# One fused attention, FFN and mixture-of-experts kernel: TensorE's program for the FFN chunks written straight instead of as a loop, and half of chunk 0's first product placed ahead of unit 4's transposes

## What is computed

```python
q_s = softmax(q, axis=-1);  k_s = softmax(k, axis=2)          # 8 x 8 heads, 576 x 64 each
x = q_s @ (k_s^T v)                                           # -> x: 4608 x 512
h = x @ w_in;  g = h - tanh(h);  x = g @ w_out                # 512 -> 2048 -> 512
logits = norm(x) @ norm(expert_emb).T / tau;  e = argmax(logits)
out = softmax(logits)[e] * (relu(x @ w1[e]) @ w2[e])          # 512 -> 1024 -> 512, by token
```

## Time and profile before

| | |
|---|---|
| median of 3 runs | 1433.05 us (1432.52 to 1435.44) |
| the profiled execution's own time | 1435.76 us |
| its span, first to last instruction | 1433.8 us |
| PE busy | 1411.8 us, 98% |
| DVE, ACT, POOL busy | 905.3, 767.2, 393.4 us |
| stages in the span | opening with chunks 0 to 15 to about 118 us; loop of slots 16 to 159 to 820.85 us; slots 160 to 191 to about 957 us; expert tiles to the end |

### The profile page before, as it was taken

How to read it: one execution, slowest core, us unless ns; L and a number is a source line. 1 busy time by engine, 2 the same in 40 slices (tenths; PEclk the granted TensorE clock), 3 DMA queues, 4 the chain that set the end, 5 groups by cost and what they waited for, 6 DMA issues and landing times.

```text
span 1433.8 us, 27060 instructions
## 1 busy us (share of the span) xinstructions
PE 1411.8 (98%) x8124; PEld 1218.9 (85%) x8125; DVE 905.3 (63%) x1761; ACT 767.2 (54%) x1574; POOL 393.4 (27%) x345
## 2 busy tenths in 40 slices
PE   7999999999999999999999999999999999999997
PEld 5888888888888888888888888888888888888886
DVE  7996888886688887578888666676323313342221
ACT  6876576766566575657676666663324223242221
POOL 4422343532243433325343323221000000001000
PEclk9999999999999999999999999999999999999999
DMA  9632022121012122002121002035411411501110
GB/s 233 179 75 65 2 72 50 50 50 50 1 48 51 52 46 51 24 1 73 30 68 26 23 1 82 0 104 170 164 44 43 155 44 33 168 29 51 44 35 33
DMA packets 132387, 90.32 MB, mean 63 GB/s; under 512 B 107160, under 2 KB 113048, under 8 KB 132128
## 3 DMA queue, kind: packets, MB, share of 16 engines
q1 hardware_dynamic: 126128, 69.49, 18.5%
q0 software_dynamic: 5840, 18.92, 3.4%
q10 hardware_dynamic: 288, 0.33, 0.1%
HBM read 69.80 MB, written 21.28 MB: 64 GB/s over the span
## 4 chain that ended last, share of the span: by engine, by line
PE 94%; DVE 2%; issue 1%; POOL 1%; ACT 1%; DMA 0%; SPq 0%; POOLq 0%; DVEq 0%; ACTq 0%
PE ps L586 28%; PE ps L587 28%; PE ps L588 28%; PE ps L803 2%; PE ps L680 2%; PE ps L772 1%; PE ps L702 1%; PE ps L686 1%; PE ps L691 1%; PE ps L722 1%; PE ps L672 0%; PE ps L643 0%; DMA q_sb<-q 0%; DVE wo_lo L1260 0%; DVE gs L1112 0%
## 5 line engine op out<-in xcount | busy, mean ns | idle before, releaser
L1550 POOL TENSOR_TENSOR g_lo<-gs,g_hi 128x384 fp32r<-128x384 f32 x191 | 195.0, 1021 | 568.2 <-ACT g_hi L908 568.0
L586 PE MATMUL ps<-x_hi,wi_hi 128*128 128x384 f32 x768 | 277.9, 362 | 1.2 <-issue 1.2
L587 PE MATMUL ps<-x_lo,wi_hi 128*128 128x384 f32 x768 | 260.0, 339 | 0.0
L588 PE MATMUL ps<-x_hi,wi_lo 128*128 128x384 f32 x768 | 259.9, 338 | 0.0
L896 ACT ACTIVATE usq<-ps 128x384 f32<-128x384 f32 x192 | 94.1, 490 | 287.1 <-PE ps L588 286.6
L586 PE MATMUL ps<-wo_hi,g_hi 128*128 128x512 f32 x570 | 225.7, 396 | 1.9 <-issue 1.9
L587 PE MATMUL ps<-wo_lo,g_hi 128*128 128x512 f32 x570 | 226.7, 398 | 0.0
L588 PE MATMUL ps<-wo_hi,g_lo 128*128 128x512 f32 x570 | 225.0, 395 | 0.0
L1109 DVE SCALAR_TENSOR_TENSOR gs<-gs,ps 128x384 f32<-128x384 f32 x192 | 105.9, 551 | 145.2 <-ACT gs L903 144.0
L1360 DVE TENSOR_TENSOR t_lo<-ps,t_hi 128x512 fp32r<-128x512 f32 x37 | 25.6, 691 | 242.6 <-ACT t_hi L998 238.2
L1112 DVE TENSOR_TENSOR gs<-gs,usq 128x384 f32<-128x384 f32 x192 | 171.6, 894 | 0.0
(11 more groups left out here) (225 smaller groups left out, 2700.0 us busy)
## 6 DMA issues: line engine op xcount, KB each, us to landing
w_raw<-w SPq DMA_DIRECT2D x10, 2048.0 KB
xrow<-scratch SPq DMA_DIRECT2D x36, 257.0 KB, 2.7
v_sb<-v SPq DMA_DIRECT2D x60, 144.0 KB, 3.4
k_sb<-k SPq DMA_DIRECT2D x56, 144.0 KB, 3.4
q_sb<-q SPq DMA_DIRECT2D x56, 144.0 KB, 3.2
in_raw<-w_in SPq DMA_DIRECT2D x8, 512.0 KB, 6.1
out_raw<-w_out SPq DMA_DIRECT2D x8, 512.0 KB, 5.8
scratch<-pad_d SPq DMA_DIRECT2D x8, 257.0 KB, 4.2
```

The lines of the kernel that those rows point to most:

```text
L586: mm(out_, a_hi, b_hi, start=first, stop=False)
L587: mm(out_, a_hi, b_lo, start=False, stop=False)
L588: return mm(out_, a_lo, b_hi, start=False, stop=last)
L1550: G.tensor_tensor(g_lo[:, (s - 1) % 3], gs[:, (s - 1) % 2], g_hi[:, (s - 1) % 3].bitcast(F32), ALU.subtract).then_inc(glo_ready, 1)
```

## The change

It has two parts, both in PE's stream alone.

1. A new item `early:0` stands in PE's order between `out:3` and `qa:4`. It runs the first product of chunk 0 for its first two groups of three matmuls (`SOONER`, units 0 and 1), waiting only for the x of units 0 and 1 and the first split piece of `w_in`. `chunk:0` then runs the other two groups (`LATER`).
2. PE no longer goes through `walk`. Slots 15 to 191 are written out one after the other, with constants in every wait. The other four engines keep their loops.

```diff
-        "qa:3 kv:3 qb:3 out:2 kT:4 out:3 qa:4 row:4 chunk:0 kv:4 qb:4 chunk:1 out:4 chunk:2 kT:5 chunk:3 "
+        "qa:3 kv:3 qb:3 out:2 kT:4 out:3 early:0 qa:4 row:4 chunk:0 kv:4 qb:4 chunk:1 out:4 chunk:2 kT:5 chunk:3 "
...
+SOONER, LATER = (0, 1), (2, 3)
...
-        def first_product(m, s):
+        def first_product(m, s, pieces=range(DC)):
...
-                pe.wait_ge(xlo_b, m * 8 + (UPB if blk == 0 else 2 * UPB) + 1)
+                units = UPB if blk == 0 else 2 * UPB
+                pe.wait_ge(xlo_b, m * 8 + units + 1 if DC - 1 in pieces else len(pieces) + 1)
...
-            pe.wait_ge(g_ready, done(m, s, -2))
+            if 0 in pieces:
+                pe.wait_ge(g_ready, done(m, s, -2))
...
-            for dc in range(DC):
+            for dc in pieces:
...
-            last.then_inc(h_ready, 1)
+            if DC - 1 in pieces:
+                last.then_inc(h_ready, 1)
...
+            if what == "early":
+                first_product(0, 0, SOONER)
+                return
...
-            first_product(0, c)
+            first_product(0, c, LATER if c == 0 else range(DC))
...
-        walk(pe, slot, {SUPER - 1: first_rows_T})
+        for c in range(FILL, NCH):
+            if c == NCH - 1:
+                first_rows_T()
+            slot(c // SUPER, c % SUPER)
```

## The result

The changed kernel takes 1429.97 us in the median of 16 runs (1428.25 to 1432.03). The kernel before, run beside it, takes 1433.85 us (16 runs, 1431.55 to 1436.75). The ratio is 0.9971, 95% interval 0.9964 to 0.9978: 0.29% less time, about 4.1 us, where 4.0 us (0.28%) were forecast. The forecast 1429.05 us started from 1433.05 us; the kernel before now has 0.8 us more, and the changed kernel 0.9 us more. The span fell from 1433.8 to 1429.8 us.

A forecast was written before the change was run, and what follows sets the result against it. The prediction took PE, busy 98% of the span, to bound the kernel. Its terms, -4.09 + 0.2 - 0.1 = -4.0 us, took 1433.05 us to 1429.05 us, 0.28% less, range 1427.9 to 1431.3 us.

The forecast's parts named there:

- The loop on PE: At the FFN loop's two back-branches on PE: writing the loop straight removes the stalls, -4.09 us.
- What is late next: Behind ACT's own back-branch: POOL's piece comes late and PE waits 0.1 us at each, +0.2 us (0 to 2.26).
- The early matmuls: Six matmuls ahead of unit 4's transposes: PE's 1.1 us lead is mostly lost to DVE, -0.1 us.
- The kept lead: Rival, opening: PE keeps the early matmuls' 1.1 us lead, 1428.1 us; chance 0.08.
- ACT's branch taking over: Rival, FFN back-branches: ACT's full 1.13 us lateness reaches PE at each, 1.9 us gained, 1431.1 us; chance 0.13.
- Removal of the stalls: Rival, straight FFN stream on PE: the change moves the stalls and does not remove them, about 1433 us; chance 0.06.
- The expert loop did not begin to fetch: Rival claimed the opposite: PE's expert loop begins to fetch, 2.04 us at each of six back-branches, 1441.3 us; chance 0.08.

The follow-up runs named there:

- straight tiles: The changed kernel with PE's expert loop (7 turns of 4 tiles) written straight too; ratio 0.9967 to the kernel before.
- All engines straight: The changed kernel with slots 15 to 191 written straight for ACT, DVE and POOL too; ratio 0.9960 to the kernel before.
- early only: The kernel before with half of chunk 0's first product ahead of unit 4's transposes, PE's loop kept; ratio 0.9999 to the kernel before.
- turn of 12 tiles: The changed kernel with PE's expert loop as 4 tiles straight, then 2 turns of 12 tiles, 2020 instructions each; ratio 0.9997 to the kernel before.
- loop four slots later: The kernel before with PE's FFN loop over slots 20 to 163 instead of 16 to 159, same body length; ratio 1.0015 to the kernel before.
- straight only: The kernel before with PE's FFN program written straight and no matmuls moved in the opening; ratio 0.9963 to the kernel before.

## Why the prediction was right

**The loop on PE, -4.09 us.** Right: the middle gained 4.11 us in the changed kernel. The experiments give the mechanism that the prediction took from two rows. A back-branch to code that is no longer in PE's instruction memory waits for a block to be fetched, 2.5 to 3.1 us in the FFN loop, less what PE has queued. It waits for a second block too, if that block's border lies close behind the loop's start. The Trainium skill's page "Runtime: NRT & Kernel Launch" (instruction fetch) says that fetch runs in blocks of 256 instructions and that PE's memory holds 2048. The runs agree with the first by the estimated 260 instructions between two transfers of the straight tiles, and with the second as a bound: 1351 stay and 2020 don't.

**What is late next, +0.2 us.** The mechanism was right and the size a little high: ACT is late behind its own back-branch, POOL's piece ends at 355.66 us, and PE starts on it at 355.82 at full pace. It measured 0 us. All engines straight has the same middle, 698.13 us.

**The early matmuls, -0.1 us.** Right in sign and place, 0.2 us in the trace and nothing that timing can tell. The experiments, compared within one kind of opening, give 0.1 to 0.2 us. I had put the limit at DVE, 0.10 us of slack. Counted from the transposes, DVE's first operation on chunk 1 came at 7.87 us before and 7.68 after. The slack was 0.19, since durations in the profile overlap the next start a little and an end worked out from them is too late. The wait for ACT's exponentials that took the first 0.67 us I had not priced.

**The sum.** By the two stretches the change gained 4.11 + 0.21 = 4.3 us, where 4.0 were forecast; both small terms were off in the same direction. The timing's 4.1 us (3.2 to 5.2) can't tell the two apart. That the span of the profiled execution is the forecast 1429.8 us to the tenth is luck: as the last section shows, such spans differ by 2 us at their end alone.

**The rivals.** The kept lead and ACT's branch taking over fall by early only and all engines straight. Removal of the stalls was complete. The expert loop did not begin to fetch: its 682 instructions are well below what stays. But the rival was a real one for a longer body, as the turn of 12 tiles shows.

## What to carry to other kernels

Where PE is busy nearly all the time, ask for its "issue" waits and set them beside the program's back-branches and the instruction queue's transfers; then compare the step over the branch with the same step elsewhere, which gives the cost before anything is changed. A loop is free as long as its turn stays in the instruction memory (1351 instructions did here, 2020 did not). One that doesn't should be written straight, or, if it must stay a loop, have a long run of queued matmuls just ahead of its back-branch and the next block's border far behind its start.
Filling an engine's gap with work from later gives only what the engines that feed it allow: here 1.1 us of filled gap became at most 0.2 us.

## What the runs showed of the hardware that I had not expected

The clock answered to two of the stalls of about 2 us: behind 1.77 us of idle time (and 12 small matmuls ahead of it) the granted clock was 0.50 for the next product, and behind 2.06 us (turns of 12 tiles) it was 0.53. Behind 1.93 us, at the second back-branch of the kernel with the loop four slots later, it stayed up. A stall of this length can thus cost some 1.7 times its own time (3.49 against 2.08 us, 3.8 against 2.2), or not.

The granted clock also differs in code that no kernel here changed, between the FFN and the tiles. From 965 to 970 us the changed kernel ran at 0.82, and straight only at 1.00 with less busy time:

```profile
965.00:970.00 5.00, 5.00 (x34) 4.12 (x33) 4.69 (x16) 2.38 (x5) 0.00 (x0) 0.82 0.00 0
```

```profile
965.00:970.00 5.00, 4.14 (x33) 3.35 (x32) 4.72 (x15) 2.54 (x5) 0.00 (x0) 1.00 0.00 0
```

Here the lower clock leaves nothing behind. By POOL's second transfer of a result row, the next mark behind this place, the changed kernel (998.01 - 817.01 = 181.00 us after chunk 160) is level with straight only (999.08 - 818.11 = 180.97 us):

```profile
998.01 0.99 POOL L1631 DMA_INDIRECT out<-osb,xrow  x1 [12.59 <-DVE osb L1503]
...
1423.16 0.98 POOL L1631 DMA_INDIRECT out<-osb,xrow  x1 [4.82 <-DVE osb L1503]
```

```profile
999.08 0.99 POOL L1631 DMA_INDIRECT out<-osb,xrow  x1 [11.39 <-DVE osb L1503]
...
1424.02 0.98 POOL L1631 DMA_INDIRECT out<-osb,xrow  x1 [4.64 <-DVE osb L1503]
```

Yet from chunk 160 to the end the changed kernel took 612.8 us of its span, straight only 610.4, and the kernel before 612.9. The second row of each pair is the last transfer of the kernel. Counted from chunk 160, it is issued within 0.24 us in the two kernels, and from its start to the end of the span it is 6.6 us in the changed kernel and 4.5 in straight only. The difference is the landing of this one transfer, 4.9 against 2.7 us from issue:

```profile
out<-osb,xrow POOLq DMA_INDIRECT x1, 4.9
```

```profile
out<-osb,xrow POOLq DMA_INDIRECT x1, 2.7
```

So the spans of single profiles differ by some 2 us for a reason outside the change, and a difference of 0.2 us can be read only from stretches like the ones used above.
